# ScalarE's copy of the next keys one step later, and three of the twelve inverse-table tiles made by ScalarE

## The chip, the cores and the metric

The kernel runs on one core of one Trainium2 chip. The metric is the device time of a run in microseconds (us). The core has five engines with instruction queues of their own: TensorE (PE in the profile), VectorE (DVE), ScalarE (ACT), GpSimd (POOL) and SyncE (SP, which here only issues transfers). They wait for each other by semaphores.

## What is computed

Three stages in a row: attention with a band of 96 keys, 8 global keys and a bias by distance; a mixture of experts with one expert for each token, where a gate decides whether a token chooses afresh or keeps its predecessor's expert; and a mixing stage over tokens and channels.

```python
# attention: B, H, S, D = 2, 8, 768, 64
scores = scale * np.matmul(q, k.transpose(0, 1, 3, 2)) + bias
scores = np.where(keep, scores, -1000000000.0)     # keep: global or local keys
a = np.exp(scores - np.max(scores, axis=-1, keepdims=True))
a = a / (np.sum(a, axis=-1, keepdims=True) + 1e-09)
x = np.matmul(a, v)                                # then heads side by side: [B, S, 512]
# experts: E = 8, F = 1024; e is the expert of token (b, s)
h = np.maximum(x[b, s] @ w1[e], 0.0)
out[b, s] = p[e] * (h @ w2[e])
# mixing
theta = x @ w_theta
y = w_tok_r @ (x * cos(theta)) + w_tok_i @ (x * sin(theta))
u = x + y
result = u + np.maximum(u @ w_ch, 0.0)
```

## The kernel before

*Attention* works on 48 pairs g = 6h + i of a head h and a tile i of 128 queries, both batches at once. The code for each engine is written out in rounds r; round r of TensorE issues the scores of pairs 2r+2 and 2r+3 (`scores`, L1255), the values of earlier pairs (`values`, L1317), the product with the gates (`turn_back`, L1280) and the transposes of the probabilities of pairs 2r and 2r+1 (`turn`, L1300). VectorE adds the bias to the scores and takes the row minimum (`bias`, the raw instructions of L959), copies transposed probabilities out of PSUM (L940, L947, L949), and in two of three rounds normalises (`normalise`: den_e, rec, part, x_tok, and at its end `add_logits`, L923, which adds `part` to `lg`; both lie in SBUF and have 54 columns). ScalarE makes the exponentials (`exponential`, L688), copies the odd pairs' probabilities (`turned`, L696) and, once a head, the first half of the attention result out of PSUM (`first_half`, outT, L681). TensorE may start the values of the next three pairs only when outT has been copied.

All products with 32-bit precision split an operand into a high and a low part. ScalarE makes the high part of the keys two heads ahead (`keys_high`, k_hi, L671, two instructions). GpSimd makes, head by head and in this order, q_hi (L606), q_lo (L609), k_lo from k_raw and k_hi (`keys_low`, L483, two instructions) and the next head's `levels` (L615). TensorE's first scores of a head wait for k_lo (`s_k_split`), GpSimd's q_hi waits for the scores of the head before, and SP's load of the keys and queries after that waits for k_lo too.

*Routing* follows attention. VectorE works out in small steps each token's slot, as a tile number and a place in the tile. `in_tile` and `at_place` hold these as 0/1 tables, `at_place` scaled with the token's number less 2048 (`NO_TOKEN`); the product of the two on TensorE (L1393, 12 matmuls, one for each tile of 128 tokens) is the inverse table: which token stands in each slot. VectorE adds 2048 (`token_at`, L1103), GpSimd gathers the first expert tile's rows with it, and TensorE starts on them (L1401). Between the inverse table and the gather TensorE runs 11 matmuls of zeros (`keep_running`, L1240; each is two in the trace). The 12 tiles of `at_place` are made by VectorE one after the other (L1095), and TensorE waits for each.

Of the kernel before, what the change touches and what calls it, by code (L numbers as in the profile page):

```python
# [18 lines left out]
ACT = mybir.ActivationFunctionType  # L19
# [6 lines left out]
P = 128  # L26
B, H, S, DH = 2, 8, 768, 64
D = H * DH
E, F = 8, 1024
PIECE = 2 * F  # L30
QT = S // P
NT = B * QT
# [2 lines left out]
SLOT_TILES = (B * S - E) // P + E  # L35
TOKENS = B * S
MAP = SLOT_TILES + 1
HALF = S // 2
REL = S + (QT - 1) * P
NARROW = slice((QT - 2) * P, (QT + 1) * P)  # L40
# [11 lines left out]
NO_TOKEN = 2048  # L52
# [8 lines left out]


_WIDTHS = [("numbers", 2), ("key_near", WINDOW), ("rel_near", NARROW.stop - NARROW.start), ("ident", P), ("before", P), ("ones", P), ("first", NT), ("erev", NT * E), ("starts", E * NT),
           ("carry", E * NT), ("place", P), ("token", NT), ("tile", NT * MAP)]
COL, _at = {}, 0
for _name, _w in _WIDTHS:
    COL[_name] = (_at, _at + _w)
# [4 lines left out]
def constants():  # L72
    t = np.zeros((P, NCONST), np.float32)
    p = np.arange(P)[:, None]
    def put(name, a):
        t[:, COL[name][0]:COL[name][1]] = a

    rel = p - np.arange(REL)[None] + (QT - 1) * P
    rel = np.where(rel >= 0, rel * FIRST_SLOPE, BIG)
    put("rel_near", rel[:, NARROW])  # L80
    put("key_near", np.arange(WINDOW)[None])
    put("ident", np.eye(P))
    put("before", p < np.arange(P)[None])
    put("ones", 1.0)
    first = np.zeros((P, NT))
    first[0, ::QT] = 1.0
    put("first", first)
    put("erev", np.tile(E - np.arange(E), NT)[None])
    put("starts", np.tile(np.where(np.arange(NT) > 0, np.arange(NT) * P, -1), E)[None])
    put("carry", np.tile(np.arange(NT) > 0, E)[None])  # L90
    put("place", np.arange(P)[None])
    put("token", p + np.arange(NT)[None] * P - NO_TOKEN)
    put("tile", np.tile(np.arange(MAP), NT)[None])
    return t, np.concatenate([rel, np.broadcast_to(np.arange(S)[None], (P, S))], axis=1).astype(np.float32)


def width(g):

    return P if g % QT == 0 else WINDOW
# [88 lines left out]
def program(nc, q2, kx, vx, w_gates, w_experts, w_theta, w_tok_rT, w_tok_iT, w_ch,  # L188
# [5 lines left out]
    with ExitStack() as ctx:  # L194
# [7 lines left out]
        def sb(name, shape, dt=F32):  # L202
            size = int(np.prod(shape[1:])) * 4
            t = nc.alloc_sbuf_tensor_at(name, shape, dt, offset=cursor[0])
            cursor[0] += -(-size // 32) * 32
            assert cursor[0] <= base + ARENA_KB * 1024, name
            return t

        def sem(name):
            return ctx.enter_context(nc.semaphore(name))  # L210
# [31 lines left out]
        s_exact = sem("exact")  # L242
        s_in_tile = sem("in_tile")
        s_at_place = sem("at_place")
        s_g_act = sem("g_act")
        s_g_dve = sem("g_dve")
        s_row_mm = sem("row_mm")
# [10 lines left out]
        s_map = sem("map")  # L258
# [55 lines left out]
        ps = ctx.enter_context(nc.psum_tensor("ps", [P, 8, 512], F32))  # L314
# [15 lines left out]
        slot = sb("slot", [P, NT], I32)  # L330
        token_at = sb("token_at", [P, 1 + MAP], U32)
        rows_in = sb("rows_in", [P, 1], U32)
# [47 lines left out]
        held = sb("held", [P, E])  # L380
        home = sb("home", [P, 2, NT])
        at_place = sb("at_place", [P, NT, P], F32R)
        in_tile = sb("in_tile", [P, NT, MAP], F32R)
        end_routing = cursor[0]

# [45 lines left out]
        def con(name):  # L431
            return cst[:, COL[name][0]:COL[name][1]]
# [230 lines left out]
        def _(act):  # L663
# [27 lines left out]
            def windows():  # L691
                def turned(g):
                    home, was = prob_home(g)
                    act.wait_ge(s_pt1, g // 2 + 1)
                    wait(act, s_av, was + 1)
                    act.copy(probT[:, home, :], ps[:, 5, :]).then_inc(s_cp1, 1)  # L696

                def exponentials(g):
                    for b in range(B):
                        act.wait_ge(s_raw, 2 * g + b + 1)  # L700
                        if g % 2:
                            wait(act, s_pt1, g // 2 - 1)
                        else:
                            wait(act, s_pt0, g // 2 - 1)
                        exponential(g, b, width(g))

                keys_high(1)
                exponentials(0)
                exponentials(1)
                for r in range(PAIRS // 2):  # L710
                    for g in (2 * r + 2, 2 * r + 3):
                        if g < PAIRS:
                            exponentials(g)
                    if r % 3 == 2:
                        first_half(2 * (r // 3))
                    if not both_by_vector(r):
                        turned(2 * r + 1)
                    if r % 3 == 1 and r // 3 + 2 < H:
                        keys_high(r // 3 + 2)

            def whole_rows():
# [14 lines left out]
                     cst[:, COL["before"][0]:COL["ones"][1]]).then_inc(s_exact, 1)  # L736
            act.wait_ge(s_g_dve, 1)
            act.activation(gate_f[:], gate_e[:], ACT.Exp).then_inc(s_g_act, 1)
            def hidden(t):
                for half, (done, high) in enumerate(((s_m_h0, s_m_r0), (s_m_h1, s_m_r1))):  # L740
                    act.wait_ge(done, t + 1)
                    act.wait_ge(s_m_y, t + 1)
                    act.activation(hT_hi[:, 4 * half:4 * half + 4, :],  # L743
                                   ps[:, 1 + half, :].rearrange("p (c q) -> p c q", c=4), ACT.Relu).then_inc(high, 1)
# [79 lines left out]
            for s in range(-2, NT):  # L824
                m, n = s + 2, s - QT
# [14 lines left out]
        def _(dve):  # L840
# [138 lines left out]
            def whole_rows():  # L979
# [3 lines left out]
                def rows_of_head(h, last):  # L983


                    for i in range(QT):
                        dve.wait_ge(s_scores, QT * h + i + 1)
                        dve.sem_inc(s_seen, 1)
                        for b in range(B):
                            dve.tensor_tensor_reduce(raw_rows[:, b, :].rearrange("p (c k) -> p c k", c=2),  # L990
                                                     ps[:, 2 * b:2 * b + 2, 0:HALF],
                                                     dist[:, i, :].rearrange("p (c k) -> p c k", c=2), -DH ** -0.5, 3.0e38,
# [43 lines left out]
            def along(a, inner):  # L1036
# [51 lines left out]
            place, slot_tile = home[:, 0, :], home[:, 1, :]  # L1088
            then(dve.tensor_scalar(slot_tile, val, (P - 1) / 2, 1 / P, ALU.subtract, ALU.mult))
            then(dve.tensor_scalar(slot_tile, slot_tile, MAGIC, MAGIC, ALU.add, ALU.subtract))  # L1090
            then(dve.scalar_tensor_tensor(place, slot_tile, -float(P), val, ALU.mult, ALU.add))
            dve.tensor_tensor(in_tile[:], con("tile").rearrange("p (n c) -> p n c", n=NT), along(slot_tile, MAP),
                              ALU.is_equal).then_inc(s_in_tile, 1)
            for n in range(NT):
                dve.tensor_scalar(at_place[:, n, :], con("place"), place[:, n:n + 1], con("token")[:, n:n + 1],  # L1095
                                  ALU.is_equal, ALU.mult).then_inc(s_at_place, 1)

            all_to = tiles_to.rearrange("p e o -> p (e o)")
# [1 line left out]
            dve.tensor_copy(first_tile[:, 0:E + 1], all_to)  # L1100
            dve.tensor_scalar(first_tile[:, E + 1:E + 2], all_to[:, E:], 1.0, None, ALU.subtract).then_inc(s_slot_ready, 1)  # L1101
            dve.wait_ge(s_inverse, 1)
            dve.tensor_scalar(token_at[:, 1:], ps[:, 3, 0:MAP], float(NO_TOKEN), None, ALU.add).then_inc(s_map, 1)  # L1103

            then(dve.tensor_reduce(total_p, gate_f[:], AX.X, ALU.add))
            then(dve.tensor_scalar(total_p, total_p, 1e-9, None, ALU.add))
# [102 lines left out]
            for s in range(-2, NT):  # L1209
                m, n = s + 2, s - QT  # L1210
# [25 lines left out]
        def _(pe):  # L1236
# [152 lines left out]

            pe.wait_ge(s_in_tile, 1)  # L1390
            for n in range(NT):
                pe.wait_ge(s_at_place, n + 1)
                last = pe.matmul(ps[:, 3, 0:MAP], at_place[:, n, :], in_tile[:, n, :], start=(n == 0), stop=(n == NT - 1))  # L1393
            last.then_inc(s_inverse, 1)
            keep_running(11, 4)
# [181 lines left out]
```

## Time and profile before

| | us |
|---|---|
| median of 3 runs | 512.64 (512.34 to 512.86) |
| the profiled execution: its own time | 513.58 |
| the profiled execution: span from first to last instruction | 510.7 |
| TensorE, VectorE, ScalarE, GpSimd busy | 492.2, 275.1, 205.5, 101.9 |
| attention, to the last L1280 | about 11 to 98.5 |
| routing, to the first expert matmul (L1414) | about 98.5 to 119.4 |

Busy shares are means over stages that differ. What the change touches lies in the first 120 us, so the stage's own rows count, not the shares of the whole.

### The profile page before, as it was taken

Reading aid. Unit: us, or ns where it says so; the run is one execution under the profiler, and the core shown is the slowest. Engines: PE = TensorE matmul, PEld = TensorE weight load, DVE = VectorE, ACT = ScalarE, POOL = GpSimd, SP = SyncE. Lnnn points to the kernel's source line nnn. Section 1 sums busy time; section 2 is a strip of 40 time slices with the busy share of each in tenths; the row PEclk is TensorE's granted clock in tenths of the full one; section 3 lists DMA queues with packets and bytes.
Section 4 is the critical chain, followed back from the end, with each engine's and each line's share of the span. In section 5 each row is a group of like instructions: output and inputs, shape, how many; then the busy total and the mean of one; then the engine's idle time right before and its main releaser. Section 6 shows DMA issues by size and latency. Waiting matters only on the chain.

```text
span 510.7 us, 9337 instructions
## 1 busy us (share of the span) xinstructions
PE 492.2 (96%) x3356; PEld 430.5 (84%) x3356; DVE 275.1 (54%) x642; ACT 205.5 (40%) x422; POOL 101.9 (20%) x113
## 2 busy tenths in 40 slices
PE   9899999759999999999999999999999999999997
PEld 8788888549999999999999999877888878888885
DVE  5688888774115141424423421778877675444243
ACT  4978887312114141414414454645553242222010
POOL 3998680011111111111111111000000000000000
PEclk9999999958999999999999999999999999999999
DMA  8645318623949283838947301050000000000012
GB/s 334 237 150 198 124 53 332 239 64 114 390 165 349 103 331 116 313 129 309 377 192 285 115 24 41 24 207 0 2 1 0 1 0 22 21 22 21 22 62 82
DMA packets 20696, 71.14 MB, mean 139 GB/s; under 512 B 2734, under 2 KB 5806, under 8 KB 16432
## 3 DMA queue, kind: packets, MB, share of 16 engines
q1 hardware_dynamic: 17872, 63.88, 33.2%
q0 software_dynamic: 2640, 6.30, 3.5%
q8 instruction: 23, 0.38, 0.3%
q10 hardware_dynamic: 144, 0.44, 0.2%
q14 instruction: 17, 0.14, 0.1%
HBM read 62.49 MB, written 10.49 MB: 143 GB/s over the span
## 4 chain that ended last, share of the span: by engine, by line
PE 84%; DVE 10%; issue 4%; ACT 2%; DVEq 0%; ACTq 0%
PE ps L1385 44%; PE ps L1414 22%; PE ps L1240 4%; PE ps L1317 3%; PE ps L1280 3%; PE ps L1300 2%; PE ps L1255 2%; PE ps L1401 1%; PE ps L1489 1%; PE ps L1450 1%; DVE raw L959 1%; ACT z_hi L810 1%; DVE z L1158 1%; DVE x_tok L1190 1%; DVE z_lo L1135 1%
## 5 line engine op out<-in xcount | busy, mean ns | idle before, releaser
L1414 PEld LDWEIGHTS ps<-xT,w_sb 128*128 128x128 f32 x1024 | 116.7, 192 | 1.8 <-DVE xT L1130 0.6
L1414 PE MATMUL ps<-xT,w_sb 128*128 128x128 f32 x1024 | 117.0, 275 | 0.4 <-DVE xT L1130 0.4
L1116 DVE SCALAR_TENSOR_TENSOR hT_lo<-ps,hT_hi 128x512 fp32r<-128x512 f32 x32 | 22.1, 690 | 98.1 <-ACT hT_hi L743 98.0
L1125 DVE TENSOR_TENSOR w_lo<-w_sb,w_hi 128x1024 fp32r<-128x1024 f32 x32 | 37.0, 1220 | 38.9 <-ACT w_hi L773 38.9
L688 ACT ACTIVATE prob<-raw,row_min 128x256 f32<-128x256 f32 (+1 forms) x96 | 45.9, 480 | 14.5 <-DVE row_min L959 14.5
L1385 PE MATMUL ps<-w_hi,hT_hi 128*128 128x512 f32 x128 | 51.2, 400 | 0.0
L1385 PE MATMUL ps<-w_lo,hT_hi 128*128 128x512 f32 x128 | 49.9, 390 | 0.0
L1385 PE MATMUL ps<-w_hi,hT_lo 128*128 128x512 f32 x128 | 49.9, 390 | 0.0
L743 ACT ACTIVATE hT_hi<-ps 128x512 fp32r<-128x512 f32 x32 | 19.1, 597 | 72.5 <-PE ps L1414 72.5
L749 ACT COPY yout<-ps 128x512 f32<-128x512 f32 x16 | 9.4, 587 | 71.1 <-PE ps L1385 71.1
L773 ACT CAST w_hi<-w_sb 128x1024 fp32r<-128x1024 f32 x32 | 31.1, 1044 | 12.5 <-DVE first_tile L1101 12.5
L959 DVE CUSTOM_DVE_ANT_0 raw<-ps,levels 128x256 f32<-128x256 f32 (+1 forms) x96 | 32.6, 394 | 2.6 <-PE ps L1255 2.6
L643 POOL DMA_INDIRECT y_rows<-yout,rows_out x16 | 16.4, 1026 | 77.5 <-ACT yout L749 77.5
L1385 PE MATMUL ps<-z_hi,wtr_hi 128*128 128x512 f32 x72 | 29.0, 403 | 0.0
L1317 PE MATMUL ps<-probT,v_sb 128*64 128x128 f32 x352 | 25.7, 281 | 3.3 <-ACT outT L681 2.0
L1385 PE MATMUL ps<-z_hi,wti_hi 128*128 128x512 f32 x72 | 28.3, 393 | 0.0
L1385 PEld LDWEIGHTS ps<-w_hi,hT_lo 128*128 128x128 f32 x128 | 24.0, 188 | 5.0
L1385 PE MATMUL ps<-z_hi,wtr_lo 128*128 128x512 f32 x72 | 28.1, 391 | 0.0
L1385 PE MATMUL ps<-z_hi,wti_lo 128*128 128x512 f32 x72 | 28.0, 389 | 0.0
L1385 PE MATMUL ps<-z_lo,wti_hi 128*128 128x512 f32 x72 | 28.0, 389 | 0.0
L1385 PE MATMUL ps<-z_lo,wtr_hi 128*128 128x512 f32 x72 | 28.0, 389 | 0.0
L1385 PEld LDWEIGHTS ps<-w_lo,hT_hi 128*128 128x128 f32 x128 | 24.1, 188 | 4.5
(178 smaller groups left out, 945.1 us busy)
## 6 DMA issues: line engine op xcount, KB each, us to landing
w_sb<-in_w_experts SPq DMA_DIRECT2D x32, 1024.0 KB, 7.9
v_sb<-in_vx SPq DMA_DIRECT2D x8, 640.0 KB, 4.1
q_raw<-in_q SPq DMA_DIRECT2D x8, 384.0 KB, 5.4
x_tok<-y_rows SPq DMA_DIRECT2D x12, 256.0 KB, 4.5
out_x<-o_sb SPq DMA_DIRECT2D x12, 256.0 KB, 2.0
k_raw<-in_kx SPq DMA_DIRECT2D x7, 432.0 KB, 4.7
x_rows<-x_tok SPq DMA_DIRECT2D x2, 1152.0 KB, 11.1
wtr<-in_w_tok_rT SPq DMA_DIRECT2D x6, 384.0 KB
```

Source lines behind the costliest of these rows:

```text
L643: pool.indirect_dma_start(y_rows, bass.IndirectOffsetOnAxis(ap=rows_out[:], axis=0), yout[:], None, bounds_check=last_row, oob_is_err=Fals ...
L688: act.activation(where, of, ACT.Exp, bias=row_min[:, m:m + 1], scale=-1.0, accum_out=den[:, h % 2 if w < S else 0, i, b:b + 1]).then_inc(s ...
L743: act.activation(hT_hi[:, 4 * half:4 * half + 4, :], ps[:, 1 + half, :].rearrange("p (c q) -> p c q", c=4), ACT.Relu).then_inc(high, 1)
L773: act.copy(w2_hi_quarter(q), quarter(w_sb, par, q)).then_inc(s_w2_hi, 1)
L959: dve.tensor_tensor_reduce(raw[:, g % 4, b * WINDOW:b * WINDOW + w], ps[:, 2 * (g % 2) + b, 0:w], levels[:, h, min(i, 1), 0:w], -DH ** -0. ...
L1116: dve.scalar_tensor_tensor(hT_lo[:, part, :], ps[:, 1 + half, :].rearrange("p (c q) -> p c q", c=4), 0.0, hT_hi[:, part, :].bitcast(F32), ...
L1125: dve.tensor_tensor(quarter(w_lo, par, q), quarter(w_sb, par, q), w2_hi_quarter(q).bitcast(F32), ALU.subtract).then_inc(s_w2_lo, 1)
L1240: pe.matmul(ps[:, bank, 0:P], blank[:], blank[:], start=True, stop=True)
L1280: last = pe.matmul(ps[:, back_bank(q), j * TURNED:(j + 1) * TURNED], outT[:, q % 2, j * P:(j + 1) * P], wg[:, q // 2, :], start=True, stop ...
L1317: last = pe.matmul(ps[b * DH:(b + 1) * DH, 6, (i % GROUP) * P:(i % GROUP + 1) * P], v_sb[:, h % 2, b, block, :], probT[:, home, b * WINDOW ...
L1385: last = pe.matmul(bank, a, b, start=(start and j == 0 and m == 0), stop=(stop and j == count - 1 and m == 2))
L1414: last = pe.matmul(ps[:, 1 + half, f * P:(f + 1) * P], w_sb[:, par, c // 2, j:j + P], xT[:, c, :], start=(c == 0), stop=(c == DC - 1))
```

## The change

ScalarE's `keys_high` of the head after next is issued in the last of a head's three rounds, behind outT and the probT copy, instead of in the middle one. And ScalarE makes tiles 9, 10 and 11 of `at_place`, in two instructions each: the absolute value of the token's place less the column number, and a relu of that times (number - 2048) plus (2048 - number). It is 2048 - number where the distance is zero, and nothing elsewhere. VectorE's nine tiles take the same sign, and `token_at` is 2048 less the product.

```diff
+BY_SCALAR = 3
+    put("from_end", NO_TOKEN - p - np.arange(NT)[None] * P)
...
-                    if r % 3 == 1 and r // 3 + 2 < H:
+                    if r % 3 == 2 and r // 3 + 2 < H:
                         keys_high(r // 3 + 2)
...
+            act.wait_ge(s_in_tile, 1)
+            for j in range(BY_SCALAR):
+                n = NT - BY_SCALAR + j
+                act.activation(distance[:, j, :], con("place"), ACT.Abs, bias=home[:, 0, n:n + 1],
+                               scale=-1.0).then_inc(s_distance, 1)
+                act.wait_ge(s_distance, j + 1)
+                act.activation(at_place[:, n, :], distance[:, j, :], ACT.Relu, bias=con("from_end")[:, n:n + 1],
+                               scale=con("token")[:, n:n + 1]).then_inc(s_at_place_act, 1)
...
-            for n in range(NT):
-                dve.tensor_scalar(at_place[:, n, :], con("place"), place[:, n:n + 1], con("token")[:, n:n + 1],
+            for n in range(NT - BY_SCALAR):
+                dve.tensor_scalar(at_place[:, n, :], con("place"), place[:, n:n + 1], con("from_end")[:, n:n + 1],
...
-            dve.tensor_scalar(token_at[:, 1:], ps[:, 3, 0:MAP], float(NO_TOKEN), None, ALU.add).then_inc(s_map, 1)
+            dve.tensor_scalar(token_at[:, 1:], ps[:, 3, 0:MAP], -1.0, float(NO_TOKEN), ALU.mult, ALU.add).then_inc(s_map, 1)
...
-                pe.wait_ge(s_at_place, n + 1)
+                if n < NT - BY_SCALAR:
+                    pe.wait_ge(s_at_place, n + 1)
+                else:
+                    pe.wait_ge(s_at_place_act, n - NT + BY_SCALAR + 1)
```

ScalarE's queue in rounds 1 and 2 of attention before the change, where the k_hi casts are those of head 2 (the words in brackets are the semaphores that an instruction waits for; line numbers are those of each file):

```order
L696 COPY probT<-ps 128x512 [waits av,pt1]
L671 CAST k_hi<-k_raw 128x6x224 [waits scores,k_in0]
L671 CAST k_hi<-k_raw 128x6x32
L688 ACTIVATE prob,den<-raw,row_min 128x128 [waits pt0,raw] x2
L688 ACTIVATE prob,den<-raw,row_min 128x256 [waits pt1,raw] x2
L681 COPY outT<-ps 128x384 [waits av]
L696 COPY probT<-ps 128x512 [waits pt1]
L688 ACTIVATE prob,den<-raw,row_min 128x256 [waits pt0,raw] x2
```

And after it:

```order
L701 COPY probT<-ps 128x512 [waits av,pt1]
L693 ACTIVATE prob,den<-raw,row_min 128x128 [waits pt0,raw] x2
L693 ACTIVATE prob,den<-raw,row_min 128x256 [waits pt1,raw] x2
L686 COPY outT<-ps 128x384 [waits av]
L701 COPY probT<-ps 128x512 [waits pt1]
L676 CAST k_hi<-k_raw 128x6x224 [waits scores,k_in0]
L676 CAST k_hi<-k_raw 128x6x32
L693 ACTIVATE prob,den<-raw,row_min 128x256 [waits pt0,raw] x2
```

The two casts moved past four exponentials, outT and one probT copy; the same happens in each head up to 5. GpSimd's order is unchanged.

ScalarE's queue in the routing after the change; before it, the first two rows are followed at once by the wait for `slot_ready`:

```order
L740 CAST exact_c<-cst 128x256 [waits c_in]
L743 ACTIVATE gate_f<-gate_e 128x96 [waits g_dve]
L748 ACTIVATE distance<-cst,home 128x128 [waits in_tile]
L751 ACTIVATE at_place<-distance,cst 128x128 [waits distance]
L748 ACTIVATE distance<-cst,home 128x128
L751 ACTIVATE at_place<-distance,cst 128x128 [waits distance]
L748 ACTIVATE distance<-cst,home 128x128
L751 ACTIVATE at_place<-distance,cst 128x128 [waits distance]
L461 UNCONDITIONAL_BRANCH [waits slot_ready]
```

Six instructions are new there, and the last three of TensorE's 12 matmuls wait for them instead of for VectorE.

## Rows read from the trace of the kernel before

**Rows 1.** Busy time of each engine in one head of attention (stretch, length, engines, clock, DMA)

```profile
39.91:50.52 10.61, 10.33 (x116) 8.59 (x115) 9.21 (x40) 8.81 (x29) 8.75 (x6) 1.00 0.44 159
```

**Rows 2.** Who waited for whom, first 130 us: total, times, longest

```profile
PE ps L1317 <- ACT outT L681: 2.0, 2, 1.5
```

**Rows 3.** Timeline of TensorE (start, us, line, operation, idle before and its releaser)

```profile
23.49 1.53 PE L1317 MATMUL ps<-probT,v_sb 128*64 128x128 f32 x24 [1.52 <-ACT outT L681]
...
29.29 0.33 PE L1255 MATMUL ps<-k_hi,q_hi 64*128 64x128 f32 x2
...
34.11 1.53 PE L1317 MATMUL ps<-probT,v_sb 128*64 128x128 f32 x24 [0.47 <-ACT outT L681]
...
39.91 0.33 PE L1255 MATMUL ps<-k_hi,q_hi 64*128 64x128 f32 x2
...
44.34 1.53 PE L1317 MATMUL ps<-probT,v_sb 128*64 128x128 f32 x24
...
82.32 0.33 PE L1255 MATMUL ps<-k_hi,q_hi 64*128 64x128 f32 x2
```

**Rows 4.** Timeline of ScalarE, heads 1 to 4

```profile
19.65 1.56 ACT L671 CAST k_hi<-k_raw 128x1344 fp32r<-128x1344 f32 x2
...
22.89 0.46 ACT L681 COPY outT<-ps 128x384 f32<-128x384 f32 x1
...
31.74 0.40 ACT L688 ACTIVATE prob<-raw,row_min 128x128 f32<-128x128 f32 x1 [0.29 <-DVE row_min L959]
...
40.02 0.59 ACT L696 COPY probT<-ps 128x512 f32<-128x512 f32 x1
40.50 1.57 ACT L671 CAST k_hi<-k_raw 128x1344 fp32r<-128x1344 f32 x2
41.97 0.40 ACT L688 ACTIVATE prob<-raw,row_min 128x128 f32<-128x128 f32 x1
...
43.73 0.46 ACT L681 COPY outT<-ps 128x384 f32<-128x384 f32 x1
44.09 0.58 ACT L696 COPY probT<-ps 128x512 f32<-128x512 f32 x1
45.66 0.51 ACT L688 ACTIVATE prob<-raw,row_min 128x256 f32<-128x256 f32 x1 [0.99 <-DVE row_min L959]
```

**Rows 5.** Timeline of VectorE around two updates of lg

```profile
30.64 0.85 DVE L923 TENSOR_TENSOR lg<-lg,part 128x54 f32<-128x54 f32 x1
31.41 0.28 DVE L959 CUSTOM_DVE_ANT_0 raw<-ps,levels 128x128 f32<-128x128 f32 x1
...
41.26 0.20 DVE L923 TENSOR_TENSOR lg<-lg,part 128x54 f32<-128x54 f32 x1
41.38 0.28 DVE L959 CUSTOM_DVE_ANT_0 raw<-ps,levels 128x128 f32<-128x128 f32 x1
...
44.63 0.65 DVE L923 TENSOR_TENSOR lg<-lg,part 128x54 f32<-128x54 f32 x1
```

**Rows 6.** Timeline of GpSimd, and the minimum, median and maximum of its k_lo

```profile
29.59 1.83 POOL L609 TENSOR_TENSOR q_lo<-q_raw,q_hi 128x768 fp32r<-128x768 f32 x1
...
42.14 3.62 POOL L483 TENSOR_TENSOR k_lo<-k_raw,k_hi 128x1344 fp32r<-128x1344 f32 x2 [1.26 <-ACT k_hi L671]
45.73 1.50 POOL L615 TENSOR_SCALAR levels<-levels 128x512 f32<-128x512 f32 x1
47.74 1.47 POOL L606 TENSOR_TENSOR q_hi<-q_raw,one 128x768 fp32r<-128x768 f32 x1 [0.52 <-PE ps L1255]
...
L483 POOL TENSOR_TENSOR k_lo<-k_raw,k_hi x14: 593/1825/3070, 14.6 to 77.0; 128x1344 fp32r<-128x1344 f32 x7, 128x192 fp32r<-128x192 f32 x7
```

**Rows 7.** Routing: two pieces of the chain that ended last; one group by tile

```profile
109.95 3.11 PE ps L1393 x12
113.06 4.89 PE ps L1240 x22
...
L1095 DVE TENSOR_SCALAR at_place<-cst,home x12: 340/341/343, 109.5 to 112.3; 128x128 fp32r<-128x128 f32 x12
```

More of the change, by code:

```diff
@@ L63 @@
 _WIDTHS = [("numbers", 2), ("key_near", WINDOW), ("rel_near", NARROW.stop - NARROW.start), ("ident", P), ("before", P), ("ones", P), ("first", NT), ("erev", NT * E), ("starts", E * NT),
-           ("carry", E * NT), ("place", P), ("token", NT), ("tile", NT * MAP)]
+           ("carry", E * NT), ("place", P), ("token", NT), ("from_end", NT), ("tile", NT * MAP)]
 COL, _at = {}, 0
@@ L244, in program @@
         s_at_place = sem("at_place")
+        s_distance = sem("distance")
+        s_at_place_act = sem("at_place_act")
         s_g_act = sem("g_act")
@@ L382, in program @@
         at_place = sb("at_place", [P, NT, P], F32R)
+        distance = sb("distance", [P, BY_SCALAR, P])
         in_tile = sb("in_tile", [P, NT, MAP], F32R)
```

## Prediction

> **What bounds the kernel now.** I read the busy time of each engine by head first. In a steady head of attention, 10.61 us long, TensorE has 10.33 us of work and VectorE 9.21 us [rows 1]. So TensorE nearly sets the pace, with 0.28 us of a head without work. Then I looked at who waited for whom: TensorE waited for outT twice, 2.0 us in all [rows 2]. In head 0 the wait is 1.52 us, in head 1 0.47 us [rows 3]; in later heads no idle time is put down to it, but L1317 starts at 44.34, 0.61 us after outT started at 43.73, just as at 23.49 (0.60 us after 22.89), so outT still releases it there [rows 3, 4]. ScalarE makes outT late, since the k_hi casts stand two instruction groups ahead of it: casts at 40.50, exponentials at 41.97, outT at 43.73 [rows 4].
>
> The last view is the one that decides: VectorE and GpSimd side by side. The small lg update on VectorE takes 0.20 us at 41.26, when GpSimd is idle. At 30.64 it takes 0.85 us: GpSimd's q_lo ran from 29.59 to 31.42, and the next VectorE instruction starts at 31.41. At 44.63 it takes 0.65 us, to 45.28: the first of the two k_lo instructions started at 42.14 and is 3.07 us long, so it ends at 45.21 [rows 5, 6]. lg adds two tensors that both lie in SBUF. It is held until the running GpSimd instruction ends; the raw instructions, which take one operand from PSUM, are not.
>
> **The move of k_hi.** The same two casts per head (1.47 us of ScalarE's time, 40.50 to 41.97) now stand behind outT and the probT copy. No instruction is added; GpSimd's k_lo, the semaphore that TensorE's next scores wait for, and the SP queue's load of the keys two heads on hang behind them.
>
> *Head 0.* The exponentials that stood behind the cast now start at 19.65, where the cast started [rows 4]. The stretch from exponentials to outT is 43.73-41.97 = 1.76 us, so outT starts at 21.41 instead of 22.89. TensorE starts its values 0.61 us later, at 22.02: a gain of 1.47 us. The exponentials behind the cast at its new place find it over: idle time of 0.99 us ended at 45.66, and the cast now ends near 45.4 at that place in a head. So on ScalarE the move itself is free.
>
> *From outT to the next lg, two ways.* TensorE's way: outT to values 0.61; values to the next head's first scores 39.91-34.11 = 5.80; scores to lg 41.26-39.91 = 1.35 [rows 3, 5]. Together 7.76 us. GpSimd's way, with the cast now behind outT: outT to probT copy 0.36 (43.73 to 44.09); copy to cast 0.48 (40.02 to 40.50); cast to k_lo 1.64 (40.50 to 42.14); k_lo to levels 3.59 (42.14 to 45.73); levels to q_hi 47.74-45.73-0.52 of idle time = 1.49; together 7.56 us [rows 4, 6]. q_hi then runs 1.47 us. So **lg arrives 0.20 us after q_hi has started, and is held until q_hi ends**, 9.03 us after outT. Before the change the same lg met an idle GpSimd (41.26), because k_lo and all behind it ran some 3.5 us earlier.
>
> *The loop this closes.* When lg is free, raw starts at once, as at 31.41; exponentials start 0.33 us later (31.74), outT 1.76 us after that [rows 4, 5]. A head then takes 9.03 + 0.33 + 1.76 = 11.12 us, against 10.60 now. outT of head 1 is at 21.41 + 11.12 = 32.53 (before: 33.50, since the values started at 34.11), and four loops later, for head 5, at 77.01. The values start at 77.62, head 7's first scores 5.80 later, at 83.42. Before they start at 82.32 [rows 3]. GpSimd has no q_hi after that, so both versions run alike from here. **This part costs 1.1 us**: 1.5 gained at first, about 0.5 lost in each of five heads. (Sums of rows rounded to 0.01 us make it 1.0 or 1.1; I take 1.0.)
>
> Two further waits stay covered. k_lo ends about 2.48+3.62 = 6.10 us after outT and the next scores come 6.41 us after it, 0.3 us to spare; were that gone, the scores would be late but lg would still wait for the same q_hi. The key and query loads that SP queues behind k_lo are issued 3 to 4 us later, and are used more than 10 us after that.
>
> The row of q_hi itself never overlaps an lg here. From below: if it does not hold lg, nothing is lost (first rival). From above: if it holds it like q_lo and k_lo do, the sum stands. I take the second, because q_hi is the same kind of instruction, an elementwise one that reads SBUF, as the two that do hold it.
>
> The Trainium skill (SBUF — State Buffer, "SBUF: two separate sides") has the rule for this: VectorE and GpSimd share a port pair under an exclusive lock, a VectorE instruction with two SBUF inputs needs it against any GpSimd instruction that reads SBUF, and whoever starts first keeps it for its whole instruction. By that rule q_hi and levels block lg as well, and the sum is the one above; by the two overlaps in the rows alone q_hi is open, and a q_hi that does not block gives the first rival's time.
>
> **The rows of the inverse table.** VectorE makes 12 at_place tiles with starts from 109.5 to 112.3, so 0.255 us each; TensorE's 12 matmuls follow at that pace, 109.95 to 113.06, and 22 fill-in matmuls of 4.89 us, still in the chain, come right behind [rows 7]. Nine tiles free VectorE 0.77 us earlier. ScalarE is idle here. Its three pairs (absolute value, then relu, 128 columns, like the 0.40 us exponential at 31.74 [rows 4]) take at most 6 x 0.40 = 2.4 us, from 109.6 to 112.0, and the first two are ready long before. TensorE still has three matmuls to do after the ninth, at its own pace: no slower than the fill-ins' 4.89/22 = 0.22 us (these move 128 columns, not 20), and at best nothing. The gain is 0.77 - 3 x 0.22 = 0.1 us up to 0.77 us. I take 0.17 us a matmul, nearer the fill-in row: **0.25 us gained**. The order shows no table load ahead of ScalarE's six instructions. The extra table of constants and the multiplication in token_at cost nothing that a row could show: same instructions, other operands. The routing chain behind moves with it, since the fill-ins start earlier by the same amount.
>
> **Sum.** +1.0 - 0.25 = +0.75 us: the profiled execution would go from a span of 510.7 to 511.45 us, and its own time from 513.58 to 514.3. The median of the runs is 512.64, 0.94 below the profiled one, and I put the change on it: **513.4 us**. Differences under 0.2%, 1.03 us, can hardly be told from none.
>
> **Rivals.**
> *lg is not held* (it slips past, or q_hi does not hold it). For: the margin is 0.20 us out of a sum of eight rows, and no row shows a q_hi against an lg. Against: both GpSimd instructions that met an lg held it; and an lg 0.2 us earlier would meet levels, and wait only to its end. With no hold at all TensorE's 10.33 us is the bound: head 2's scores at 29.29-1.47 = 27.82 [rows 3], head 7's at 27.82 + 5 x 10.33 = 79.47, which is 2.85 us sooner. With the routing that is -3.1 us: 509.5. If only some heads escape, between 509.5 and 512.4. Together 0.26.
> *Slower: lg misses q_hi's end and stays behind q_lo too.* q_lo starts right after q_hi and runs 1.83 us [rows 6], so one such miss costs 1.9 us, +2.65 in all, 515.3; five of them some 10 us. It decides from the first miss. Against: at 45.2 lg got in between two k_lo instructions that follow each other without a gap. 0.06.
> *The routing part gives nothing or 0.77*, or the loop is 0.05 us longer or shorter per head (0.25 us in all): inside the forecast's own range, 512.9 to 514.2.
>
> **Chances and range.** Forecast as told 0.62; lg not held, in part or always, 0.26; held by q_lo too 0.06; something else 0.06. The forecast's own range is 512.9 to 514.2; about a quarter of it lies over +1.03 us. So slower 0.155 + 0.05, about 0.20; faster needs most of the holds gone, 0.24; the same 0.56. The range goes down to 509.8, which takes in most of the first rival, and up to 514.3.
>
> **What the new profile would show.** TensorE's 1.52 us wait for outT gone, values of head 0 near 22.0. lg after the first scores of heads 2 to 6 some 1.3 to 1.5 us long, each ending with q_hi, and the lg that was 0.65 us back at 0.2. Scores of head 7 near 83.4. k_lo some 3.5 us later in each head. The last inverse matmul 0.25 us nearer to in_tile. I am wrong if those lg rows read 0.2 us; then the head takes about 10.3 us and the kernel is faster. I am also wrong if TensorE waits for k_lo, or for ScalarE's three tiles.

## The result: 0.5% slower, outside the forecast range

| kernel | median, us | lowest to highest | ratio to before, 95% interval |
|---|---|---|---|
| before, same chip | 512.92 | 512.28 to 514.57 (8 runs) | |
| changed | 515.51 | 514.2 to 518.13 (8 runs) | 1.0049, 1.0028 to 1.007 |
| changed, second time, other runs | 515.69 | 512.96 to 517.69 (12 runs) | 1.0044, 1.0025 to 1.0064 |

The profiled run took 515.69 us with a span of 513.7; before it was 513.58 and 510.7. The change cost 2.3 to 2.6 us where 0.75 was forecast.

### The profile page after: what moved, and what is told of

It reads as the page before. It is cut to its first block, busy times and chain, and to the rows that moved or that the text cites. A ratio compares the mean times of both kernels' runs of the same rounds, so it can differ in the third digit from the quotient of the medians.

```text
span 513.7 us, 9340 instructions
## 1 busy us (share of the span) xinstructions
PE 492.7 (96%) x3356; PEld 431.0 (84%) x3356; DVE 276.8 (54%) x639; ACT 207.2 (40%) x428; POOL 101.9 (20%) x113
## 4 chain that ended last, share of the span: by engine, by line
PE 86%; DVE 6%; issue 3%; ACT 2%; DMA 2%; SPq 0%; DVEq 0%; POOLq 0%; ACTq 0%
PE ps L1400 44%; PE ps L1432 22%; PE ps L1332 4%; PE ps L1315 3%; PE ps L1270 3%; PE ps L1255 3%; PE ps L1295 2%; PE ps L1419 1%; DMA xin<-x_rows,token_at 1%; PE ps L1507 1%; PE ps L1468 1%; ACT prob L693 1%; ACT z_hi L825 1%; DMA x_rows<-x_tok 1%; DVE z L1173 1%
## 5 line engine op out<-in xcount | busy, mean ns | idle before, releaser
L1432 PEld LDWEIGHTS ps<-xT,w_sb 128*128 128x128 f32 x1024 | 116.7, 192 | 1.8 <-DVE xT L1145 0.6
L488 POOL TENSOR_TENSOR k_lo<-k_raw,k_hi 128x1344 fp32r<-128x1344 f32 (+1 forms) x14 | 25.4, 1835 | 14.4 <-ACT k_hi L676 14.4
```

The lines of the kernel that those rows point to most:

```text
L488: last = eng.tensor_tensor(low, whole, high.bitcast(F32), ALU.subtract)
L1432: last = pe.matmul(ps[:, 1 + half, f * P:(f + 1) * P], w_sb[:, par, c // 2, j:j + P], xT[:, c, :], start=(c == 0), stop=(c == DC - 1))
```

## The profile after

VectorE's timeline of the changed kernel (start, us, line, operation), beside [rows 5]:

```profile
29.72 1.33 DVE L938 TENSOR_TENSOR lg<-lg,part 128x54 f32<-128x54 f32 x1
30.98 0.28 DVE L974 CUSTOM_DVE_ANT_0 raw<-ps,levels 128x128 f32<-128x128 f32 x1
...
40.82 1.31 DVE L938 TENSOR_TENSOR lg<-lg,part 128x54 f32<-128x54 f32 x1
42.05 0.28 DVE L974 CUSTOM_DVE_ANT_0 raw<-ps,levels 128x128 f32<-128x128 f32 x1
...
44.83 0.21 DVE L938 TENSOR_TENSOR lg<-lg,part 128x54 f32<-128x54 f32 x1
```

GpSimd's timeline in the same stretch, beside [rows 6]:

```profile
29.49 1.50 POOL L611 TENSOR_TENSOR q_hi<-q_raw,one 128x768 fp32r<-128x768 f32 x1
...
40.58 1.47 POOL L611 TENSOR_TENSOR q_hi<-q_raw,one 128x768 fp32r<-128x768 f32 x1
42.13 1.84 POOL L614 TENSOR_TENSOR q_lo<-q_raw,q_hi 128x768 fp32r<-128x768 f32 x1
46.62 3.07 POOL L488 TENSOR_TENSOR k_lo<-k_raw,k_hi 128x1344 fp32r<-128x1344 f32 x1 [2.65 <-ACT k_hi L676]
```

q_hi starts at 40.58, the lg update at 40.82, 0.24 us later, and it lasts until 42.13, where q_hi gives way to q_lo. So it reads 1.31 us instead of 0.20, in each of the five heads 2 to 6 (29.72, 40.82, 51.90, 62.97, 74.05). The other lg is back at 0.21.

TensorE's timeline, beside [rows 3], and one head's busy times, beside [rows 1]:

```profile
22.57 1.53 PE L1332 MATMUL ps<-probT,v_sb 128*64 128x128 f32 x24
...
33.67 1.53 PE L1332 MATMUL ps<-probT,v_sb 128*64 128x128 f32 x24 [0.83 <-ACT outT L686]
...
44.74 1.53 PE L1332 MATMUL ps<-probT,v_sb 128*64 128x128 f32 x24 [0.83 <-ACT outT L686]
...
83.77 0.33 PE L1270 MATMUL ps<-k_hi,q_hi 64*128 64x128 f32 x2
```

```profile
39.46:50.54 11.08, 10.21 (x115) 8.67 (x115) 9.78 (x40) 8.71 (x29) 8.35 (x6) 1.00 0.40 137
```

The wait of 1.52 us in head 0 is gone, and each of the next five heads (1 to 5) has one of 0.83 us in its place. The head is 11.08 us long instead of 10.61, and VectorE's "busy" time has grown by 0.57 with no instruction added: the held lg counts as busy though it only waits.

The chain that ended last has a new link behind attention, beside [rows 7]:

```profile
115.05 5.42 DMA xin<-x_rows,token_at
120.47 0.04 issue
120.51 0.67 PE ps L1419 x4
```

The gathered rows land 5.42 us after the issue. TensorE's fill-in matmuls are over by then; it sits idle for 1.13 us. In the kernel before it went from the fill-ins straight on.

*The 3.0 us between the two profiled spans*, stretch by stretch (starts of the same instruction in both): start to head 0's first scores +0.55 (11.34, then 11.89); from there to head 7's first scores +0.90 (70.98, then 71.88); to in_tile +0.16; in_tile to token_at -0.13 (3.97, then 3.84); token_at to the expert stage's xT +1.19 (5.53, then 6.72); the rest +0.33 (392.07, then 392.40). The +0.55 is chance: over all the profiles below, changed or not, the first scores come between 10.77 and 12.10 us. The +1.19 understates what late rows cost, since 5.53 is long for the kernel before: in its three later profiles this stretch takes 5.0 to 5.1 us, and in the later profiles of the changed kernel 5.0 to 5.2, or 6.7 where the rows are late.

## The experiments

**The two parts alone.** In the changed kernel the move is one condition:

```diff
-                    if r % 3 == 1 and r // 3 + 2 < H:
+                    if r % 3 == 2 and r // 3 + 2 < H:
                         keys_high(r // 3 + 2)
```

move_alone is the kernel before with this line; tiles_alone is the changed kernel without it.

> Only the k_hi casts are moved. If the hold of lg behind q_hi is the cause in attention, this kernel shows lg rows of 1.3 us in heads 2 to 6, a head of 11.1 us, head 7's first scores about 1.3 us later than before, and a time 1.0 to 1.5 us over the kernel before. If the rest of the loss (about 1.3 us between the gather's issue and its landing) belongs to the three tiles, it is absent here; if it comes by chance or from the later start, it shows here too and the time is 2.5 us over.

> Only the three at_place tiles by ScalarE. Attention must read as before (head of 10.6 us, one lg of 0.65 us a head). Forecast by the routing term as measured in the changed kernel: last inverse matmul 0.1 us nearer to in_tile, time 0 to 0.3 us under the kernel before. Rival: ScalarE's part makes the gather land later, so that TensorE waits for it about 1.1 us behind the fill-in matmuls; then the time is about 1 us over.

move_alone: 514.03 us, 1.0014 (1.0 to 1.0027), against 513.22. Its lg rows are those of the whole change:

```profile
39.82 1.32 DVE L923 TENSOR_TENSOR lg<-lg,part 128x54 f32<-128x54 f32 x1
```

Heads are 11.07 us long. tiles_alone: 512.79 us, 0.999 (0.9977 to 1.0003); lg as before. VectorE makes nine tiles and ScalarE three (group by tile; minimum, median, maximum in ns, first and last start):

```profile
L1110 DVE TENSOR_SCALAR at_place<-cst,home x9: 337/339/341, 109.7 to 111.8; 128x128 fp32r<-128x128 f32 x9
L751 ACT ACTIVATE at_place<-distance,cst x3: 493/493/493, 110.3 to 111.9; 128x128 fp32r<-128x128 f32 x3
```

So the parts are worth +0.8 and -0.4 us, +0.4 together, and the whole is +2.3 to +2.6. The mechanism of the move stands; some 2 us appear only when both parts are in. The intervals are 1.3 to 2.2 us wide, so by the times alone this remainder could be 1 us or 3.

**Is lg held by whatever GpSimd instruction runs?** The next four put lg updates elsewhere. The first two issue every lg one round later, behind the four raw instructions of the next pairs, in the changed kernel and in the one before:

```diff
-                add_logits(q, half)
+                if q >= LAST - 1:
+                    add_logits(q, half)
+                else:
+                    pending.append((q, half))
...
+                    while pending:
+                        add_logits(*pending.pop(0))
```

> The changed kernel, with VectorE's lg update of a round issued one round later, behind that round's four raw instructions, so that nothing on the path waits for it. Port hold theory: the first lg of a head now arrives about 1.1 us later, near the end of q_hi, is held 0.2 us at most, and its hold no longer delays raw; the head falls from 11.1 us to between 10.2 and 10.5 us and the time by 3 to 4 us against the changed kernel, to about 1 us under the kernel before. Rival, that late k_hi and k_lo themselves set the 11.1 us (scores waiting for k_lo, outT waiting for ScalarE): the head stays near 11.1 us and the time within 0.5 us of the changed kernel.

> The kernel before with the same later lg. Port hold theory: the first lg of a head, before free at 1.35 us after the head's scores, now comes at about 2.5 us, when k_lo (3.06 us long, begun 2.2 us after the scores) has just started, so it reads 2.5 to 2.9 us and delays the next copy on VectorE; the head grows by 1 to 2.5 us, the time by 5 to 12 us over the kernel before. Rival, that lg is slowed by something else (its own latency, a semaphore): the later place gives a little or nothing, time within 1 us of the kernel before or faster.

both_lg_late: 530.07 us, 1.0315 (1.0294 to 1.0335). 3 to 4 us less were expected, and it is 15 us more. VectorE and GpSimd:

```profile
48.24 2.63 DVE L938 TENSOR_TENSOR lg<-lg,part 128x54 f32<-128x54 f32 x1
```

```profile
47.74 3.05 POOL L488 TENSOR_TENSOR k_lo<-k_raw,k_hi 128x1344 fp32r<-128x1344 f32 x1 [5.73 <-ACT k_hi L676]
```

The first lg of a head was freed from q_hi, but the head's second one was moved as well, from a free place into k_lo (47.74 + 3.05 = 50.79; the lg ends at 50.87). I had looked only at the first. The 15 us need not all be the hold: in this kernel alone TensorE's clock falls to 1.2 GHz inside attention, in five stretches of 20.5 us together, one of them here:

```profile
42.50:52.70 10.20, 7.97 (x97) 6.59 (x98) 9.15 (x31) 6.53 (x22) 4.96 (x3) 1.00 0.24 74
52.70:56.10 3.40, 3.40 (x19) 3.09 (x16) 1.29 (x7) 2.01 (x8) 3.32 (x3) 0.50 0.62 220
```

(Stretch, length, busy time of TensorE, its weight loads, VectorE, ScalarE and GpSimd, granted clock, DMA.) No run separates the two costs.

before_lg_late: 522.15 us, 1.0155 (1.0128 to 1.0181), as expected: there the first lg meets k_lo, 2.90 us in each head, and a head takes 12.39 us.

Then only one lg of a head is moved: the first (`q % 2 == 0`) in the changed kernel, the second in the kernel before.

> The changed kernel with only the first of a head's two lg updates issued later, behind the next four raw instructions; the second stays, where GpSimd is idle. Port hold theory: the first lg comes when q_hi is about to end (held at most 0.2 us), the second finds GpSimd idle, the head falls from 11.1 us to 10.3 to 10.5, head 7's first scores 2.5 to 4 us earlier than in the changed kernel, the time 2 to 4 us under it. Rival, that the loop over k_hi and k_lo is what lasts 11.1 us: no change of the head.

> The kernel before with the second lg of a head issued later. It then comes at about 6.2 us after the head's scores, while GpSimd is in levels, an instruction with one tensor input, that runs from 5.8 to 7.3 us. If levels holds lg like the others, lg reads 0.8 to 1.2 us and the time is 1 to 4 us over the kernel before; if an instruction with one input does not hold it, lg reads 0.2 us and the time is 1 to 2 us under it.

both_even_late: 511.88 us, 0.9963 (0.9948 to 0.9978). before_odd_late: 511.85 us, 0.9976 (0.996 to 0.9992). Both beat both kernels. VectorE, then GpSimd, of both_even_late:

```profile
41.04 1.81 DVE L938 TENSOR_TENSOR lg<-lg,part 128x54 f32<-128x54 f32 x1
...
52.34 0.64 DVE L938 TENSOR_TENSOR lg<-lg,part 128x54 f32<-128x54 f32 x1
```

```profile
40.95 1.83 POOL L614 TENSOR_TENSOR q_lo<-q_raw,q_hi 128x768 fp32r<-128x768 f32 x1
...
51.09 1.82 POOL L614 TENSOR_TENSOR q_lo<-q_raw,q_hi 128x768 fp32r<-128x768 f32 x1
```

The lg is still held, now by q_lo: 1.81 us in one head, 0.64 in the next, where 0.2 us at most was expected. But raw has gone ahead of it, so less hangs on it, and heads take 10.17 and 11.29 us by turns instead of the 10.3 to 10.5 expected. In before_odd_late the second lg comes just as k_lo ends and levels begins:

```profile
46.16 0.40 DVE L923 TENSOR_TENSOR lg<-lg,part 128x54 f32<-128x54 f32 x1
```

```profile
42.30 3.61 POOL L483 TENSOR_TENSOR k_lo<-k_raw,k_hi 128x1344 fp32r<-128x1344 f32 x2 [1.38 <-ACT k_hi L671]
45.87 1.50 POOL L615 TENSOR_SCALAR levels<-levels 128x512 f32<-128x512 f32 x1
```

levels runs until 47.37, and lg, 0.29 us behind its start, is over at 46.56. It is the same in three more heads (35.81, 56.51 and 66.89, 0.39 to 0.42 us each, always 0.28 or 0.29 us behind the start of levels). So levels, which reads one tensor, did not hold lg to its end; why lg takes 0.40 us there and not 0.20 is open.

**Who holds lg can be changed.** move_alone with GpSimd's levels issued ahead of k_lo and not behind it, so that GpSimd's queries come earlier against lg:

```diff
-                pool.wait_ge(s_k_hi, h + 1)
-                keys_low(pool, h)
                 if h + 1 < H:
                     pool.wait_ge(s_level, h)
                     pool.tensor_scalar(levels[:, h + 1], levels[:, h], SLOPE_RATIO, None, ALU.mult).then_inc(s_level, 1)
+                pool.wait_ge(s_k_hi, h + 1)
+                keys_low(pool, h)
```

> The k_hi move alone, with GpSimd's levels issued before k_lo, in its idle time there. Counting busy time this helps GpSimd. By the port hold theory q_hi then ends before the first lg comes and q_lo (1.83 us) is running instead, from 6.1 to 7.6 us q_hi, 7.6 to 9.5 us q_lo after outT with lg at 7.8; lg reads about 1.7 to 1.9 us, the head 11.5 us instead of 11.1, the time about 2 us over the move alone. Rival, that q_hi alone or the length of GpSimd's chain matters: the head gets shorter by up to 0.7 us.

517.95 us, 1.0079 (1.0055 to 1.0103), heads of 11.5 us. By the ratios that is 3.3 us over move_alone where 2 were expected: five heads longer by 0.4 us make 2, and three of its four runs also have the lower mean clock, 0.983, which none of move_alone's twelve has. q_lo holds lg from 41.84 (VectorE, then GpSimd):

```profile
41.84 1.73 DVE L923 TENSOR_TENSOR lg<-lg,part 128x54 f32<-128x54 f32 x1
```

```profile
41.69 1.81 POOL L609 TENSOR_TENSOR q_lo<-q_raw,q_hi 128x768 fp32r<-128x768 f32 x1
```

This is the case of my slower rival: lg comes 0.15 us after q_lo has started, and 1.3 us of hold become 1.7.

**Where are the other 2 us?** Profiles of the whole change:

> The changed kernel as it is, once more. The two halves alone came to +0.8 and -0.4 us, the whole to +2.6. If the rest was the gather of one profile and chance, the median now is 0.3 to 1.2 us over the kernel before and the gather lands 3.7 us after its issue. If it is of the changed kernel (its code or its place in time), the gather again lands more than 5 us after its issue with late packets at the end, and the median is 2 us or more over.

> The changed kernel as it stands, for its profile. The two profiles of it so far differ from the gather on: in one the gathered rows came 5.42 us after the issue and TensorE waited 1.13 us for them (span 513.7), in the other within 3.9 us, with no wait (span 512.1). Theory A, a gather that is often late in this kernel makes the 2 us that the two parts alone do not add up to: a gather of about 5.4 us again, and a span of 513 to 514. Theory B, the late gather is a chance of one run and the 2 us lie elsewhere: a gather of 3.4 to 3.9 us, and a span over 512.5 all the same, with the surplus in the stretch from the first scores to the inverse table or behind the gather.

> The same kernel and the same two theories: A, the gathered rows about 5.4 us after the issue and a span of 513 to 514; B, 3.4 to 3.9 us after it, and whatever the span has over 511.5 lies elsewhere.

> The same kernel and the same two theories once more: A, the gathered rows about 5.4 us after the issue and a span of 513 to 514; B, 3.4 to 3.9 us after it, and whatever the span has over 511.5 lies elsewhere.

| run | span | mean clock | gather issued | first turn_x | idle before it | first to second xT |
|---|---|---|---|---|---|---|
| changed | 513.7 | 0.987 | 115.05 | 120.51 | 1.13 | 9.43 |
| changed_again | 512.1 | 0.986 | 115.13 | 119.00 | 0 | 9.43 |
| changed_look3 | 515.1 | 0.983 | 115.02 | 120.45 | 1.46 | 10.98 |
| changed_look4 | 510.9 | 0.987 | 114.06 | 117.77 | 0 | 9.43 |
| changed_look5 | 511.7 | 0.986 | 114.70 | 118.69 | 0 | 9.43 |

In two of five the rows land 5.4 us after the issue; in the others they are there by 3.7 to 4.0 us after it, when TensorE comes to them. The two late ones are the two long spans, as theory A has it, though the longer one, 515.1, lies over its 513 to 514. changed_again fits neither of its two forecasts: its median is 2.3 us over before, but the rows of its profile came in time. So the lateness belongs to single executions.

The DMA packets of the trace show what is late. The gather is 80 packets of the queue q0. In both late profiles a transfer of 16 KB on the queue q8, which the profile calls "instruction", starts just before they are all through. The changed kernel from 117 to 119.2 us, then from 119.2 to 120.4:

```profile
q0 software_dynamic: 74, 0.24, 38.3%
q8 instruction: 1, 0.02, 2.8%
```

```profile
q0 software_dynamic: 3, 0.01, 4.2%
```

Three packets start just before 117 and 74 more by 118.42; q8 runs from 118.30 to 119.27; the last three packets start at 119.26 and later. In changed_look3 77 start by 118.35, q8 runs from 118.26 to 119.22, and three start from 119.20 on. The gather's last packet ends 4.99 and 4.96 us after the issue in these two, and 3.32 to 3.59 us after it in the profiles of all other runs, changed or not; there q8 runs before the gather, over its first 0.5 us, or starts only when the gather's last 4 KB packet has started. So by the trace the late rows are three packets that waited for a load of instructions. Why it falls there in some executions and not in others, no run shows. In three of the four profiles of the kernel before it starts at 118.3 to 119.1, 1.4 us or more behind the gather's end (116.8 to 117.2); the changed kernel's gather ends at 117.4 or later, which may be all that brings the two together; that is argued, not tested.

And changed_look3 shows a second cost. Its TensorE (timeline, then clock by stretches: length, busy time of TensorE, its weight loads, VectorE, ScalarE and GpSimd, granted clock, DMA):

```profile
114.35 4.65 PE L1255 MATMUL ps<-blank 128*128 128x128 f32 x22
120.45 0.66 PE L1419 MATMUL ps<-cst,xin 128*128 128x128 f32 x4 [1.46 <-DMA xin<-x_rows,token_at]
120.95 0.61 PE L1255 MATMUL ps<-blank 128*128 128x128 f32 x4
121.99 2.29 PE L1432 MATMUL ps<-xT,w_sb 128*128 128x128 f32 x9 [0.43 <-DVE xT L1145]
```

```profile
118.00:120.00 2.00, 1.00 (x7) 0.81 (x6) 0.00 (x0) 0.00 (x0) 0.00 (x0) 0.89 0.08 20
120.00:122.00 2.00, 1.11 (x9) 0.92 (x9) 0.75 (x2) 0.00 (x0) 0.18 (x1) 0.97 0.00 0
122.00:124.00 2.00, 2.00 (x9) 2.00 (x10) 2.00 (x2) 0.00 (x0) 1.78 (x1) 0.50 0.00 0
124.00:126.00 2.00, 2.00 (x15) 2.00 (x14) 2.00 (x3) 0.00 (x0) 0.00 (x0) 0.68 0.47 131
```

TensorE had come up to 2.4 GHz at 118.45, stood idle for 1.46 us and 0.43 us, and then the grant was 0.50, 1.2 GHz, when the expert matmuls began, from 121.86 to 125.28. That stretch took 1.55 us longer (10.98 instead of 9.43). Of all 23 runs of the changed kernel, timed or profiled, seven have a mean clock of 0.983, with spans of 514.1 to 516.0; the other sixteen, at 0.986 and 0.987, lie from 510.7 to 514.2.

For the test TensorE gets more cover: 17 matmuls of zeros behind the inverse table, not 11.

```diff
-            keep_running(11, 4)
+            keep_running(17, 4)
```

> The changed kernel with 17 matmuls of zeros behind the inverse table instead of 11 (34 in the trace instead of 22): TensorE has work for 0.11 us x 12 = 1.3 us longer at the full clock. If the 2 us are the late gather and what TensorE's idleness makes of it, no run shows the half clock again behind 120 us: the runs of a mean clock of 0.983 and spans of 514 to 516 are gone or rare, a late gather costs nothing beyond the fill-ins, and the spans lie together at 512.5 to 514, with a median time of about 515 us, a little under the changed kernel's 515.6. If the fill-ins have nothing to do with it, every run is 1.3 us longer: a median of about 516.9, with spans up to 517.

> The kernel before with 17 matmuls of zeros behind the inverse table instead of 11: up to 1.3 us more work at the full clock. If the runs of the kernel before at a mean clock of 0.983 (about a third, spans of 511.1 to 512.1 against 509.9 to 511.0) are also those in which TensorE idles for late rows and falls back to half clock, they are gone here, and the median rises by only 0.7 to 1.0 us, to about 514.0. If the rows are nearly always in time in the kernel before and its lower mean clock is from elsewhere, the runs at 0.983 stay and the median rises by the whole 1.3 us, to 514.5.

changed_fill17: 514.46 us, 1.0029 (1.0016 to 1.0041). With more work it is 1.1 us *faster* than the changed kernel (515.5 to 515.7), no run of twelve is at 0.983, and the longest span is 514.0. Each against its own runs of before, 1.0029 and 1.0044 to 1.0049, that is 0.8 to 1.0 us, with intervals that overlap. before_fill17: 514.05 us, with spans of 511.4 to 512.0 at 0.987 and 512.4 to 513.2 at 0.982 and 0.983, against 509.7 to 510.9 and 511.1 to 511.9 of the kernel before beside it: 1.1 to 1.3 us longer at either clock, and six of twelve runs still at the lower one. Its median is only 0.2 us over before (513.83; 1.0008, 0.9995 to 1.002), since the times of the kernel before beside it exceed their spans by more than its own do. So the same edit costs 1.2 us of span before the change and saves 0.9 us of span after it (mean spans 511.04 and 512.24, then 513.62 and 512.73): the six matmuls recover some 2 us there by the spans, 1.1 to 1.5 by the median times. Whether they do it as cover alone is open: in both profiles with 17 matmuls the q8 transfer runs ahead of the gather (from 114.25 and 114.39), so the edit may also have moved it out of the gather's way.

Does the kernel before have late rows too?

> The kernel before, for its profile. In its one profile the last fill-in of TensorE ends at 117.7 us, when the gathered rows have been there for some time. About a third of its runs have a mean clock of 0.983 and spans of 511.1 to 512.1, the others 509.9 to 511.0. Theory A, the late gather is common to both kernels: a run at 0.983 shows rows that land 5.4 us after the issue, TensorE idle over 1 us, or half clock again behind 120 us, and a span near 511.6. Theory B, only the changed kernel has it: rows in time, and the 0.983 of this kernel is lost elsewhere, in a rise of the clock that comes later in the start or in the fill-ins.

> The kernel before and the same two theories: A, at a mean clock of 0.983 the rows land 5.4 us after the issue or TensorE is at half clock again behind 120 us; B, the rows are in time, and the lower mean clock is from another stretch.

> The kernel before and the same two theories once more: A, at a mean clock of 0.983 the rows land 5.4 us after the issue or TensorE is at half clock again behind 120 us; B, the rows are in time, and the lower mean clock is from another stretch.

Spans of 510.4, 510.2 and 510.0; the first turn_x comes 3.79, 3.85 and 3.83 us after the issue with no idle time. None of them was at 0.983, so they decide nothing on that. The profile of before_fill17 was, and shows what its 0.983 is: the clock falls earlier, at the start of routing, and not once more behind the gather: it is at 1.2 GHz from 101.6 to 118.7 us, in before from 104.4 to 118.0. tiles_alone, whose attention is that of the kernel before, was profiled at 0.983 too and shows the same (101.6 to 118.7). So the same mean clock has another cause in these than in changed_look3, which is at 1.2 GHz from 104.8 to 118.5 and then again from 121.9. Clock by stretches, before_fill17 and then before:

```profile
100.00:102.00 2.00, 0.00 (x0) 0.00 (x0) 1.83 (x10) 0.69 (x2) 0.00 (x0) 0.90 0.01 4
102.00:104.00 2.00, 0.82 (x4) 0.23 (x4) 1.18 (x5) 0.00 (x0) 0.00 (x0) 0.50 0.03 8
```

```profile
102.00:104.00 2.00, 0.35 (x4) 0.10 (x2) 1.68 (x7) 0.00 (x0) 0.32 (x1) 1.00 0.03 8
104.00:106.00 2.00, 0.92 (x4) 0.85 (x4) 0.81 (x3) 0.00 (x0) 0.20 (x1) 0.60 0.67 203
```

**The best version.** One more keeps the move and the late first lg and leaves out ScalarE's tiles; one adds cover to both_even_late.

> The keys' copy moved as in the change, no tiles by ScalarE, and the first logits update of a head issued one round later. The version with the tiles as well ran in 511.88 us, 0.9963 of before, with heads of 10.17 and 11.29 us by turns. If the tiles are worth the 0.13 us between the last inverse row and the table that the profiles show and nothing else, this one is 0.1 to 0.4 us slower than that version: 512.0 to 512.3 us. If the tiles by ScalarE are what brings the 2 us that the whole change has over its two parts (something that they upset behind the table once the heads end later), this one is faster than that version: about 510 us. Heads of 10.2 and 11.3 us by turns in both cases.

> The version with both parts and a head's first logits update one round later (511.88 us), now with 14 matmuls of zeros behind the inverse table instead of 11: 0.65 us more work at the full clock. Four of its eight runs had the mean clock 0.983, at spans of 509.7 to 510.2 against 508.6 to 510.0. If the cover helps here as in the changed kernel, the runs at 0.983 are gone and the median stays at 511.5 to 512.0; if the late rows cost this version nothing, it is 0.6 us longer, 512.5.

move_even_late: 511.75 us, 0.9973 (0.9959 to 0.9986). both_even_fill14: 512.13 us, 0.9969 (0.9956 to 0.9982). Neither can be told from both_even_late or before_odd_late; all four are 0.2 to 0.4% under the kernel before. So the tiles bring nothing here that can be measured, and by themselves they take no 2 us either. Here the cover costs 0.25 us for 0.65 us of work, a difference inside the spread of the runs.

## Why the prediction was wrong

*Head 0's gain: right.* The values start 22.57 - 11.89 = 10.68 us after the first scores; before 23.49 - 11.34 = 12.15. That is the 1.47 us forecast.

*lg held by q_hi in five heads: right.* The margin of 0.20 us, summed from eight rows, measured 0.24; a head is 11.08 us, not 11.12.

*The move costs 1.0: right against the one profile of before, on the high side against others.* From first scores to head 7's it takes 71.9 to 72.0 us with the move, and 70.98 without. But in the three later profiles of before it takes 71.31 to 71.41: there the first scores come at 10.8 to 11.0, and head 2's lg is held 1.2 to 1.3 us by q_lo (from 30.27 to 31.57 in before_look2, q_lo from 29.68). So the cost is 0.5 to 1.0, and 0.8 in the times of move_alone.

*The tiles gain 0.25: right in sign, too large.* in_tile to token_at went from 3.97 to 3.84 us. I put TensorE's own pace at 0.17 us per matmul; the 12 matmuls take 2.99 us instead of 3.11, and the last three start 0.22 us apart, the bound that gave 0.1. ScalarE's three pairs took 111.18 to 113.74, 2.56 us, against at most 2.4 (the relu takes 0.49 us, not 0.40), and their last tile was ready 0.43 us before its matmul.

*"The routing chain behind moves with it": this step failed*, and with it the sum: +0.75 us was forecast, and +2.3 to +2.6 measured. I had followed the chain only to the end of the fill-ins, as if the gather behind them were sure to be in time, and put what follows at nothing. In [rows 7] the fill-ins are the link that ends last, and I read no margin between their end and the landing of the rows. Nor are the fill-ins of one length. The 4.89 us were run at a granted clock of 0.50, up to 118.04 us; in move_alone the clock is up at 116.7, the 22 fill-ins take 4.02 us, and TensorE waits even for rows that land 3.70 us after their issue:

```profile
118.30 0.66 PE L1401 MATMUL ps<-cst,xin 128*128 128x128 f32 x4 [0.38 <-DMA xin<-x_rows,token_at]
```

In the whole change the rows land late in some runs (5.4 us after the issue, not 3.7), TensorE waits 1.1 to 1.5 us, and in one of the two profiles it loses its clock again for 1.55 us more. Shown: both effects in profiles, with token_at to xT at 6.7 us instead of 5.0 to 5.2; that the late rows are three packets behind an instruction load in both; and that six more matmuls of zeros give back 1 to 2 us there and nothing in the kernel before. This is of the size of the 2 us by which the whole passes its parts. Not shown: in how many of the unprofiled runs the rows were late, and so that this is all of the 2 us; and why it should need both parts. The issue is no later in the late runs (115.02 and 115.05, against 115.13 in time), and each part alone has only one profile, in which the rows came within 3.7 us (move_alone) and 4.2 us (tiles_alone). Also open are the 0.3 us behind xT in every profile with ScalarE's tiles; in tiles_alone they build up by 0.03 us with each tile of tokens of the expert stage.

*The range.* Its upper end, 514.3, came from the loop and the tile term alone. A cover that is just long enough should have had a term of its own, with a bound.

## To carry to other kernels

- A small VectorE update of two SBUF tensors costs what the GpSimd instruction costs that it meets. Before moving anything, lay both engines' starts side by side for one whole loop, and do it for each such update of the loop: both_lg_late freed one and ran the other into k_lo.
- An instruction with much behind it goes ahead of one that may be held: with raw ahead of the first lg of a head the changed kernel went from some 515.6 to 511.9 us, although the lg was held for 1.81 us in every other head.
- Where filler work covers a transfer, compare its end with the landing in several profiles, not with the one in hand. Here fill-ins that ended 4.65 us after the issue (17 matmuls) went with shorter runs than those that ended 3.98 to 4.32 us after it in the late profiles, for a landing at 3.7 to 5.4 us. The same filler also shrinks when the clock comes up earlier: 4.02 us in move_alone, 4.89 in before.

## What the runs showed that I had not expected

- VectorE's lg (two SBUF inputs) waited for q_hi, q_lo and k_lo to their ends, but slipped in beside levels (0.39 to 0.42 us in four heads; at 46.16, levels until 47.37). The Trainium skill (SBUF — State Buffer, "SBUF: two separate sides") has a VectorE instruction with two SBUF inputs wait for any GpSimd instruction that reads SBUF; the three elementwise ones agree (1.31, 1.81 and 2.63 us), the four rows with levels do not.
- The same gather took 5.42 and 5.39 us from issue to landing in two profiles of one kernel, and at most 3.71, 3.87 and 3.99 in three others. In the two, and in no other profile, a 16 KB load of instructions lay on the gather's end, and three of its 80 packets started only when that was over.
- Idle time of 1.46 and 0.43 us, right after the clock had come up, was followed by 1.2 GHz for the first 3.3 us of the expert stage; with 1.13 and 0.43 us in the first profile of the changed kernel the clock stayed at 2.4 GHz.
